# A fused attention and two-expert-layer kernel: the order of the instructions in its steps 2 to 4 is rewritten

## The reference

```python
def _attn_ref(q, k, v, mem_k, mem_v):          # B=4, H=8, S=768, D=64
    chunk, left_ctx, right_ctx = (32, 16, 8)   # 8 memory keys
...
        k_full = np.concatenate([mem_k, k_ctx], axis=2)
        v_full = np.concatenate([mem_v, v_ctx], axis=2)
        scores = scale * np.matmul(q_c, k_full.transpose(0, 1, 3, 2))
        a = softmax(scores)
        out[:, :, c_start:c_end] = np.matmul(a, v_full)

def _moe_ref(x, w_in, w_out, g_ln):            # x 3072x512, w_in 512x1024
    h = x @ w_in
    solu = h * softmax(h)
    ln = (solu - mean(solu)) / sqrt(var(solu) + 1e-6) * g_ln
    return ln @ w_out

def _moe2_ref(x, w_gate, w_output_gate, w1, w2):   # 8 experts, top 1
    e_idx = argmax(x @ w_gate)
    y = relu(x @ w1[e_idx]) @ w2[e_idx]            # 512 -> 1024 -> 512
    return softmax(x @ w_gate)[e_idx] * sigmoid(x @ w_output_gate)[e_idx] * y
```

## Time and profile before

| what | us |
|---|---|
| three runs, median | 714.47 |
| their lowest and highest | 713.83, 715.95 |
| the profiled execution | 716.45 |
| its span, first to last instruction | 714.8 |
| TensorE busy in the span | 679.0 |
| VectorE, ScalarE, GpSimd busy | 480.5, 349.8, 181.5 |

### The profile page before, as it was taken

How to read it: one execution, slowest core, us unless ns; L and a number is a source line. 1 busy time by engine, 2 the same in 40 slices (tenths; PEclk the granted TensorE clock), 3 DMA queues, 4 the chain that set the end, 5 groups by cost and what they waited for, 6 DMA issues and landing times.

```text
span 714.8 us, 16009 instructions
## 1 busy us (share of the span) xinstructions
PE 679.0 (95%) x4932; PEld 582.7 (82%) x4933; DVE 480.5 (67%) x777; ACT 349.8 (49%) x783; POOL 181.5 (25%) x376
## 2 busy tenths in 40 slices
PE   3898989999999999999999999999999999999985
PEld 2677888989989989989987877888888888888873
DVE  5686688888888888887736556337665748483332
ACT  3555466656656656655424444325362636352220
POOL 3121333643411111111301323122222313132221
PEclk9998999999999999999999999999999999999998
DMA  9917578788676676642254859526878677732320
GB/s 315 330 37 202 130 204 223 192 222 202 164 191 150 161 190 150 161 125 77 62 178 132 251 163 270 127 78 170 239 183 228 190 207 199 197 89 78 86 61 22
DMA packets 65699, 118.58 MB, mean 166 GB/s; under 512 B 8702, under 2 KB 41726, under 8 KB 65536
## 3 DMA queue, kind: packets, MB, share of 16 engines
q1 hardware_dynamic: 43872, 84.62, 43.7%
q10 hardware_dynamic: 15840, 16.52, 9.8%
q0 software_dynamic: 5952, 16.98, 7.6%
HBM read 73.78 MB, written 14.09 MB: 123 GB/s over the span
## 4 chain that ended last, share of the span: by engine, by line
PE 85%; DVE 5%; DMA 3%; ACT 3%; issue 2%; SPq 1%; ACTq 1%; POOLq 0%; DVEq 0%
PE banks L1414 76%; PE banks L1450 3%; PE banks L1432 2%; PE banks L1563 2%; ACT prob L697 1%; DMA r_quads<-r_sb 1%; DMA prob_quads<-prob 1%; DMA q_sb<-q_t 1%; DVE uT_lo L1020 1%; DVE hmax L1037 1%; ACTq L814 1%; DVE banks L1025 1%; DVE e_sb L1044 0%; DVE smax L997 0%; PE banks L1586 0%
## 5 line engine op out<-in xcount | busy, mean ns | idle before, releaser
L1414 PE MATMUL banks<-slots_hi_lo,rT_hi 128*128 128x512 f32 x464 | 147.3, 399 | 2.3 <-DVE rT_lo L1228 1.9
L1414 PE MATMUL banks<-slots_hi_lo,xsT_hi 128*128 128x512 f32 x464 | 124.5, 390 | 2.1 <-DVE xsT_lo L1218 1.9
L1414 PEld LDWEIGHTS banks<-slots_hi_lo,xsT_hi 128*128 128x128 f32 x464 | 86.7, 188 | 21.1 <-issue 3.2
L1414 PEld LDWEIGHTS banks<-slots_hi_lo,rT_hi 128*128 128x128 f32 x464 | 85.6, 190 | 19.9 <-issue 2.9
L1414 PE MATMUL banks<-slots_hi_lo,rT_lo 128*128 128x512 f32 x232 | 91.4, 394 | 0.0
L1414 PE MATMUL banks<-wout_hi,uT_hi 128*128 128x264 f32 x384 | 81.7, 294 | 2.0 <-DVE uT_lo L1020 2.0
L1414 PE MATMUL banks<-wout_hi,uT_lo 128*128 128x264 f32 x384 | 78.5, 286 | 0.0
L1414 PE MATMUL banks<-wout_lo,uT_hi 128*128 128x264 f32 x384 | 78.3, 286 | 0.0
L1228 DVE TENSOR_TENSOR rT_lo<-banks,rT_hi 128x1024 fp32r<-128x1024 f32 x29 | 35.5, 1224 | 58.4 <-ACT rT_hi L825 56.9
L1218 DVE TENSOR_TENSOR xsT_lo<-banks,xsT_hi 128x512 fp32r<-128x512 f32 x30 | 20.7, 689 | 77.2 <-ACT xsT_hi L785 77.2
L1414 PE MATMUL banks<-slots_hi_lo,xsT_lo 128*128 128x512 f32 x232 | 71.6, 390 | 0.0
(11 more groups left out here) (179 smaller groups left out, 1166.9 us busy)
## 6 DMA issues: line engine op xcount, KB each, us to landing
raw_w<-experts SPq DMA_DIRECT2D x56, 512.0 KB, 4.1
r_quads<-r_sb ACTq DMA_DIRECT2D x104, 128.0 KB
u_quads<-u_sb SPq DMA_DIRECT2D x88, 128.0 KB, 3.4
v_sb<-v_win SPq DMA_DIRECT2D x24, 384.0 KB, 5.1
k_sb<-k_win SPq DMA_DIRECT2D x22, 384.0 KB, 3.8
prob_quads<-prob SPq DMA_DIRECT2D x63, 128.0 KB, 3.8
x_rows<-x SPq DMA_DIRECT2D x24, 264.0 KB, 2.1
q_sb<-q_t SPq DMA_DIRECT2D x24, 256.0 KB, 3.4
```

The source lines that it names most:

```text
L1414: ins = mm(o, lhs, rhs(part, k, n), start=(k == first and lhs is not None and part == 0 and parts == (0, 1)), stop=(k == final and parts = ...
```

## The change

It changes only the order in which instructions are issued; none is added and none left out. SyncE's and GpSimd's lists stay as they are.

- VectorE: turn_u(1), low_u(1) and turn_p(3) go ahead of mask and maximum of block 4, low_x(3) ahead of copy_logits(0). Block 5's maximum goes behind weigh_h(3), h_max(3) ahead of low_u(2). Mask and maximum of block 6 go into step 4, at its start. In step 4 h_max(4) and low_u(3) now stand ahead of turn_p(5), and weigh_probs(6) goes from ahead of weigh_h(4) to behind copy_logits(2).
- ScalarE: the exponentials of block 4 and of block 5 are issued in one go each; block 4's behind square_u(2) and high_x(3), block 5's behind high_x(4) and centre_h(3). In step 4 exp_h(4) and scale_y(2) go ahead of the exponentials of block 6.
- TensorE: scores(6) go from ahead of step 4 to between the second and the third chunk of product_in(4).

```diff
--- before.py
+++ after.py
@@ -766,9 +766,9 @@
             def step(s):
                 if isinstance(s.i, int) and s.i == 4:
                     high_u(s + -1)
+                    exp_h(s)
+                    scale_y(s + -2)
                     exp_units(s + 2)
-                    scale_y(s + -2)
-                    exp_h(s)
                 else:
                     if (s + 2).within(NBLK):
                         exp_units(s + 2)
@@ -859,17 +859,15 @@
             high_u(At(0, 1))
             scale_y(At(0, 0))
             centre_h(At(0, 2))
-            exp_units(At(0, 4), range(0, 6))
+            square_u(At(0, 2))
             high_x(At(0, 3))
-            exp_units(At(0, 4), range(6, NU))
-            square_u(At(0, 2))
+            exp_units(At(0, 4))
             high_u(At(0, 2))
             exp_h(At(0, 3))
             scale_y(At(0, 1))
-            exp_units(At(0, 5), range(0, 4))
             high_x(At(0, 4))
-            exp_units(At(0, 5), range(4, NU))
             centre_h(At(0, 3))
+            exp_units(At(0, 5))
             square_u(At(0, 3))
             walk_a(act, step)
             last = At(0, NBLK - 1)
@@ -1093,11 +1091,12 @@
 
             def step(s):
                 if isinstance(s.i, int) and s.i == 4:
+                    mask_scores(s + 2)
+                    top_scores(s + 2)
                     turn_u(s + -1)
+                    h_max(s)
+                    low_u(s + -1)
                     turn_p(s + 1)
-                    low_u(s + -1)
-                    h_max(s)
-                    weigh_probs(s + 2)
                 else:
                     turn_p(s + 1)
                     if (s + 2).within(NBLK):
@@ -1113,6 +1112,8 @@
                 weigh_h(s)
                 low_x(s + 1)
                 copy_logits(s + -2)
+                if isinstance(s.i, int) and s.i == 4:
+                    weigh_probs(s + 2)
                 if (s + 3).within(NBLK):
                     mask_scores(s + 3)
                     top_scores(s + 3)
@@ -1256,27 +1257,25 @@
             weigh_probs(At(0, 3))
             low_w_out(7)
             h_max(At(0, 2))
-            mask_scores(At(0, 4))
-            top_scores(At(0, 4))
             turn_u(At(0, 1))
             weigh_h(At(0, 2))
             low_u(At(0, 1))
             turn_p(At(0, 3))
+            mask_scores(At(0, 4))
+            top_scores(At(0, 4))
+            low_x(At(0, 3))
             copy_logits(At(0, 0))
-            low_x(At(0, 3))
             weigh_probs(At(0, 4))
             turn_u(At(0, 2))
             mask_scores(At(0, 5))
-            top_scores(At(0, 5))
+            h_max(At(0, 3))
             low_u(At(0, 2))
-            h_max(At(0, 3))
             turn_p(At(0, 4))
             weigh_h(At(0, 3))
+            top_scores(At(0, 5))
             low_x(At(0, 4))
             copy_logits(At(0, 1))
             weigh_probs(At(0, 5))
-            mask_scores(At(0, 6))
-            top_scores(At(0, 6))
             walk_a(dve, step)
             last = At(0, NBLK - 1)
             rank_early()
@@ -1518,7 +1517,12 @@
 
             def step(s):
                 a, b, c = s + 1, s, s + -1
-                product_in(b, range(KD))
+                if isinstance(s.i, int) and s.i == 4:
+                    product_in(b, range(0, 2))
+                    scores(a + 1)
+                    product_in(b, range(2, KD))
+                else:
+                    product_in(b, range(KD))
                 product_out(c + -1, range(HALF, KF))
                 attention(a)
                 if (a + 2).within(NBLK):
@@ -1640,7 +1644,6 @@
             product_out(At(0, 1), range(HALF, KF))
             attention(At(0, 4))
             product_out(At(0, 2), range(0, HALF))
-            scores(At(0, 6))
             walk_a(pe, step)
             last_b = At(0, NBLK - 1)
             product_in(last_b, range(KD))
```

## The result

The new kernel takes 724.15 us (median of 4 runs, 722.6 to 724.81), the kernel before beside it 715.21 (713.83 to 718.44): ratio 1.0115, 95% interval 1.0076 to 1.0154. It is slower, by 8.9 us where no change was forecast, and outside the range.

A forecast was written before the change was run, and what follows sets the result against it. TensorE, busy 95% of the span, was taken as the bound; attention 6 starting 1.1 us early carries to the end: 716.45 - 1.1 = 715.35, forecast as 715.3 us, no change that can be told, range 711.9 to 717.7.

The forecast's parts named there:

- From prob 6 to attention 6 are 12.44 us: Block 6's weights to attention 6: weights done at 96.4, the same 12.4 us of links, attention 6 at 108.8.
- GpSimd's load comes 1 to 5 us earlier each time and is off the path: In the sum: GpSimd's earlier expert loads were taken to cost nothing, while SyncE issues the same transfers in order.
- The term for block 4's landing: Before attention 4: block 4's last weight transfer lands at 74.4, 75.1 at most; attention 4 at 76.5 after 1.7 us of wait.
- the chain of the prediction: Start to attention 6: attention 3 at 62.45, attention 4 at 76.5, block 6's weights at 96.4, attention 6 at 108.8.
- The third rival: Behind attention 6: clock falls after the longest wait, 2.8 us lost, 718.1 us, or 716.8 if in part of runs; chance 0.24.
- The wait for uT_lo: Block 1's second product: TensorE's wait of 1.75 us at 59.44 disappears, as the row's low part ends near 59.05.
- The argument that an order which keeps the clock up gains nothing over an execution that kept it: Clock at 62.5: if earlier runs mostly lacked the fall, old attention 6 at 106.7, the new order later by 2.1 us.
- Low_x does hold block 6's weights: Step 4 on VectorE: low_x of block 5 ends at 94.9, block 6's weighting follows from 95.05 to 96.4.
- the expected gain: Start of kernel: attention 4 is 2.4 us early, attention 5 is 2.3, and 1.1 us is left at attention 6.

The follow-up runs named there:

- i4: g3 with VectorE's step 4 alone ordered as in the changed kernel, ScalarE's as before: 718.97 us, ratio 1.0045.
- i3: g3 with ScalarE's step 4 alone ordered as in the changed kernel, VectorE's as before: 717.58 us, ratio 1.0028.
- i1: The changed kernel with GpSimd's third expert load held until block 4's u rows have landed: 718.78 us, ratio 1.0053.
- i2: g3 with GpSimd's third expert load issued as soon as block 4's u is centred: 716.43 us, ratio 1.0002.
- f1: The changed kernel run again, unedited, in a second set of executions: 720.97 us, ratio 1.0067.
- e4: The changed kernel with GpSimd's first expert load held until block 4's weights have landed: 716.30 us, ratio 1.0011.
- h2: The changed kernel with block 2's store and block 4's u transfers ahead of block 6's weights on SyncE's queue: 724.09 us, ratio 1.0115.
- g2: The kernel before with GpSimd's first expert load held until block 4's weights have landed: 715.80 us, ratio 0.9998.
- e2: The kernel before with the new step 4 and block 6's scores within its product, steps 2 and 3 as before: 719.91 us, ratio 1.0049.
- e1: The changed kernel with step 4 and the place of block 6's scores as before, so new steps 2 and 3 alone: 715.61 us, ratio 0.9990.
- f4: e1 with GpSimd's first expert load held until block 4's weights have landed: 713.18 us, ratio 0.9965.
- g3: The changed kernel with ScalarE's and VectorE's step 4 as before and the first expert load held until block 4's weights landed: 713.16 us, ratio 0.9964.
- e3: The changed kernel with 24 zero matmuls, 64 rows by 64 columns, ahead of each of the waits before attention 4 and 6: 731.03 us, ratio 1.0204.
- h1: The changed kernel with full-width zero matmuls, 24 ahead of the wait before attention 4 and 80 before attention 6: 727.3 us, ratio 1.0171.

## Why the prediction was wrong

**What failed.** "From prob 6 to attention 6 are 12.44 us, and every link of them is in the new kernel too." Every link is there, but one more ends last now: the landing of block 4's u rows. The prediction costed the move of block 6's weighting behind weigh_h, low_x and copy_logits for what it delays, and not for what it brings forward: u is centred 2.7 us earlier on the trace's scale, and with it square, root and GpSimd's load (1.65 us earlier), while SyncE's transfers of u stay behind those of block 6's weights and go out 1.09 us later. i4 has this with VectorE's order alone, i3 with ScalarE's alone does not. The gap of 4.5 us that kept the two apart went to 1.8. "GpSimd's load comes 1 to 5 us earlier each time and is off the path" is the same mistake in the sum (the three loads come 5.6, 0.3 and 1.7 us earlier): the load is off the path, what it moves beside is on it. It cost 1.4 us (13.86 against 12.44; i1 and i2 show it in both directions).

**The term for block 4's landing was too small.** The prediction saw that expert 0's first load would come beside block 4's transfers and took 75.1 as the bound. It measured 6.0 us for the last one where 5.2 was the upper end, VectorE began at 75.30, which is 75.9 on the scale of before (the profiled execution of after has its attention 1 0.59 us earlier, so 0.59 is added), and attention 4 was at 78.0 instead of 76.5. The prediction had a wait of 1.7 us there and no clock lost behind it; it was 3.21, and half clock followed (0.55 from 78.5 to 82.3). Counted from attention 3, attention 4, weights 6 and attention 6 were forecast at 14.1, 34.0 and 46.4 us; they came at 15.6, 36.9 and 50.8. The 4.4 us in all are 1.5 for the landing, 1.5 for the clock behind attention 4 (TensorE is done with y of block 2 15.3 us after attention 4 in the kernel after and in f1, 13.8 in e4, h2 and i1, which have the same order and no fall there) and 1.4 for the u rows. With the load held back (e4, attention 3 at 61.89) they are at 13.8, 34.0 and 46.5, and the median is 716.3, ratio 1.0011, where 715.3 had been forecast. So the chain of the prediction was right for a kernel without the two collisions. e4 still has the half clock behind attention 6, which the forecast time did not hold.

**The clock.** The third rival, a fall behind attention 6, came true, at 1.5 us rather than its 2.8; the fall behind attention 4, which cost another 1.5, no rival had. Adding up at attention 7, between the two profiled executions: weights 6 1.25 later, 1.42 for the u rows, 1.54 for the clock, 4.2 us. The other 1.7 us between the spans come at 422 us; why the wait there is longer is open. The medians differ by more in the first set (8.9 us) and by less in the second (5.2), and what the other executions lost is not shown.

**What was right.** The wait for uT_lo is gone (its subtraction ends at 58.67, 59.26 on before's scale, forecast 59.05), though 0.88 us stay, for scale_y of block 0, which I had overlooked as the next to end last. Attention 3 is at 62.4 on before's scale, forecast 62.45, after its transposition waited for the landing; the clock is at 1.00 from 62.5 to 69.5. The argument that an order which keeps the clock up gains nothing over an execution that kept it fits what was measured: in g2 and e2 the old order of steps 2 and 3 has attention 4 at 76.1 on the scale of before (76.3 was estimated), g2 attention 6 at 107.4 (106.7), and e1, the steps 2 and 3 that should have brought the gain, has the time of before. How many of before's own executions kept the clock is not shown. Low_x does hold block 6's weights: it ends at 97.19, and their first operation begins at 97.22.

**Where the expected gain went.** Counted from attention 1, attention 4 and attention 6 in e1 are 2.3 and 3.0 us earlier than in the profiled execution of before, but 0.5 later and only 0.3 earlier than in g2, which had no half clock there; the median of e1 shows no gain. With the load held back as well, f4 and g3 are 2.5 us (0.35%) faster than before: the better version is steps 2 and 3 of the change, step 4 as before on VectorE and ScalarE, and the first expert load behind block 4's weights.

## What to carry to other kernels

An operation that is moved ahead pulls everything behind it forward, background loads on another queue included: list for each moved producer which transfers it releases on every queue, and what is in flight at that moment. A transfer whose producer is early but whose queue is kept busy loses the distance to loads that are not in that queue. And before an idle time is counted as a gain, ask whether the other executions of the kernel had it.

## What the runs showed of the hardware

- A load of 512 KB on GpSimd's queue, issued within 1.8 us of the first of four transfers of 128 KB on SyncE's, goes with a landing of the last of these after 5.3 to 6.4 us in all nine profiled executions that have it, against 3.5 to 4.1 in the other eleven. i1 and i2 show that the load is the cause: behind seven transfers back to back without it, the last one lands after 4.1 us (i1).
- TensorE's granted clock fell to 0.50 while TensorE was busy without a gap with e3's fillers of 64 rows and 64 columns, and stayed at 1.00 over h1's 80 of full width (9.78 us). Why is not shown.
- The half clock behind attention 6 cost 1.5 us (14.92 us to attention 7 against 13.39), as did that behind attention 4 (15.3 against 13.8 us to y of block 2).
- The length of a wait does not alone decide on the fall. Behind attention 6 it fell after 1.90 us (i1), 2.14 (e4) and 2.77 (after), and not after 2.96 (i2). The Trainium skill ("TensorE: Matmul & The Clock Gate", section "HAM oscillation — how this bites in real kernels") asks for a longer idle time than the waits of 1.82 and 2.77 us behind which the kernel after lost the clock; the rows disagree. What decides is open.
